# Batch 0's sequence transform by cosine and sine sums, with a compact state and two tables moved

## The reference

```python
# 1. linear attention with decay lam, in blocks of the sequence
intra = (q k^T * Dmask) v ;  inter = (q * lam_pow) kv_state
kv_state = lam_block * kv_state + (k * rev_pow)^T v
# 2. Fourier mixing, normalisation, two-layer network
X = np.fft.fft(np.fft.fft(x, axis=1), axis=2)
u = x + np.real(X)
un = (u - mean(u)) / sqrt(var(u) + 1e-6)
x = u + np.maximum(un @ w_ch1, 0) @ w_ch2
# 3. gated projection
out = (sigmoid(causal_conv5(x)) * (x @ w_val)) @ w_out
```

## Time and profile before

| | us |
|---|---|
| median of three runs | 458.87 (458.79 to 459.09) |
| the profiled execution | 459.72 |
| its span | 457.9 |
| TensorE busy | 438.7 (96%) |
| VectorE busy | 268.2 (59%) |
| ScalarE busy | 151.9 (33%) |
| GpSimd busy | 147.0 (32%) |

### The profile page before, as it was taken

How to read it: one execution, slowest core, us unless ns; L and a number is a source line. 1 busy time by engine, 2 the same in 40 slices (tenths; PEclk the granted TensorE clock), 3 DMA queues, 4 the chain that set the end, 5 groups by cost and what they waited for, 6 DMA issues and landing times.

```text
span 457.9 us, 7070 instructions
## 1 busy us (share of the span) xinstructions
PE 438.7 (96%) x2892; PEld 420.1 (92%) x2892; DVE 268.2 (59%) x419; ACT 151.9 (33%) x284; POOL 147.0 (32%) x99
## 2 busy tenths in 40 slices
PE   6799859999999999999999999999999999999997
PEld 5688749989999999999999999999999999889985
DVE  1657993566835974643533424966565557999220
ACT  1154343065322141111524217344125134525312
POOL 1432536235523222332376422332422450600000
PEclk9899979999999999999999999999999999999999
DMA  6977810050220220202022022022022020001112
GB/s 209 320 219 269 289 67 2 1 183 20 73 94 0 93 77 16 92 1 94 1 93 92 1 92 94 0 93 92 1 92 93 0 93 2 0 1 70 69 47 92
DMA packets 14032, 37.05 MB, mean 81 GB/s; under 512 B 1576, under 2 KB 3120, under 8 KB 14000
## 3 DMA queue, kind: packets, MB, share of 16 engines
q1 hardware_dynamic: 14000, 36.60, 23.8%
HBM read 33.44 MB, written 3.15 MB: 80 GB/s over the span
## 4 chain that ended last, share of the span: by engine, by line
PE 87%; DVE 7%; DMA 3%; ACT 1%; issue 1%; SPq 1%; DVEq 0%
PE ps L550 10%; PE ps L552 9%; PE ps L573 9%; PE ps L572 9%; PE ps L571 9%; PE ps L551 9%; PE ps L489 3%; PE ps L657 2%; PE ps L656 2%; PE ps L655 2%; PE ps L433 2%; PE ps L408 2%; PE ps L634 2%; PE ps L635 2%; PE ps L636 2%; PE ps L444 2%
## 5 line engine op out<-in xcount | busy, mean ns | idle before, releaser
L741 ACT ACTIVATE hh<-ps 128x384 fp32r<-128x384 f32 x64 | 31.5, 492 | 173.1 <-PE ps L552 173.1
L1017 DVE SCALAR_TENSOR_TENSOR hl<-ps,hh 128x384 fp32r<-128x384 f32 x64 | 35.3, 556 | 83.3 <-ACT hh L741 83.3
L550 PE MATMUL ps<-cen_h,w1h_a 128*128 128x384 f32 x128 | 44.1, 344 | 0.5 <-DVE hl L1017 0.5
L550 PE MATMUL ps<-cen_h,w1h_b 128*128 128x384 f32 x128 | 44.2, 345 | 0.0
L552 PE MATMUL ps<-cen_h,w1l_b 128*128 128x384 f32 x128 | 43.1, 337 | 0.0
L552 PE MATMUL ps<-cen_h,w1l_a 128*128 128x384 f32 x128 | 43.1, 337 | 0.0
L573 PE MATMUL ps<-hh,w2l_b 128*128 128x384 f32 x128 | 43.1, 337 | 0.0
L572 PE MATMUL ps<-hl,w2h_b 128*128 128x384 f32 x128 | 43.1, 337 | 0.0
L571 PE MATMUL ps<-hh,w2h_b 128*128 128x384 f32 x128 | 43.1, 337 | 0.0
L551 PE MATMUL ps<-cen_l,w1h_a 128*128 128x384 f32 x128 | 43.1, 337 | 0.0
L551 PE MATMUL ps<-cen_l,w1h_b 128*128 128x384 f32 x128 | 43.0, 336 | 0.0
(11 more groups left out here) (179 smaller groups left out, 1045.5 us busy)
## 6 DMA issues: line engine op xcount, KB each, us to landing
raw_a<-in_mlp SPq DMA_DIRECT2D x16, 512.0 KB, 4.8
raw_b<-in_mlp SPq DMA_DIRECT2D x16, 512.0 KB, 4.4
chunks<-in_qkv SPq DMA_DIRECT2D x12, 512.0 KB, 5.5
chunks<-in_qkv SPq DMA_DIRECT2D x22, 256.0 KB, 4.9
out<-out_sb SPq DMA_DIRECT2D x12, 256.0 KB, 2.0
raw_a<-in_val SPq DMA_DIRECT2D x2, 512.0 KB, 4.5
raw_b<-in_out SPq DMA_DIRECT2D x2, 512.0 KB, 4.6
seq_c<-const_seq SPq DMA_DIRECT2D x1, 768.0 KB, 5.8
```

The costliest lines, as they stand in the source:

```text
L550: mm(bank, wh_, xh, start=r == 0, stop=False)
L741: nc.scalar.activation(hh[:, slot, j], ps[j][:, 0:TB], ACT.Relu).then_inc(s_hh, 1)
L1017: stt(hl[:, slot, j], ps[j][:, 0:TB], 0.0, hh[:, slot, j].bitcast(F32), ALU.max, ALU.subtract).then_inc(s_hl, 1)
```

## The change

Batch 0 takes the same way as batch 1: `seq_tile` and `add_u` go, `seq_pair` and `add_pair` take the batch as an argument. The butterfly's four instructions of `two_pairs` become `two_even` and `two_odd`, and the pieces stand at other chunks. The state holds only its 64x64 blocks, so that `fold_state` is one instruction and `from_state` twice as many, each on a quarter of the array. Hidden transforms 6 and 7 and their radix4 stand among the tiles, 8 and 9 behind the mean, and 10 and 11 in the network's steps. Weight group 0 is loaded at n=3. Its first half is cast at n=3 and subtracted at n=4, the second half after the attention. `mirror(0)` on ScalarE, which waits for the butterfly, stands at n=9 in place of n=8. At the start SP issues only keys and queries of chunk 0 ahead of the powers' write, then the keys, the decay table and the values.

```diff
-            load_chunk(0)
+            load(0, 0, 2, s_tin)
             sp.wait_ge(s_pow, 2 + 7)
             sp.dma_start(rv_dram, rv).then_inc(s_rv, 16)
-            load(1, 0, 2, s_tin)
+            load(0, 2, 3, s_kin)
             sp.wait_ge(s_rv, 16)
             sp.dma_start(decay[:, :, :], ...)
+            load(0, 3, 4, s_vin)
+            load(1, 0, 2, s_tin)
...
                 load_chunk(n)
-                if n == 4:
-                    sp.dma_start(seq_c[:, :], seq_tab[:, 0:LOW_TAB]).then_inc(s_seq, 16)
+                if n == 3:
+                    load_group(0, 0)
                 if n == 5:
-                    sp.dma_start(seq_up[:, :], seq_tab[:, LOW_TAB:]).then_inc(s_seq, 16)
+                    sp.dma_start(seq_c[:, :], seq_tab).then_inc(s_seq, 16)
+                if n == 8:
                     sp.dma_start(cw[:, :, :], conv_w).then_inc(s_cw, 16)
-                if n in (9, 10):
-                    load_group(0, 0, (n - 9,))
```

TensorE:

```diff
                 for hp in range(HP):
-                    mm(out_bank(n)[:, hp * P:(hp + 1) * P], state[:, n % NC % 2, hp, :], qd[:, n % 2, hp, :], ...)
+                    for par in range(2):
+                        rows = slice(par * Dh, (par + 1) * Dh)
+                        mm(out_bank(n)[rows, hp * P:(hp + 1) * P], state[rows, n % NC % 2, hp, :],
+                           qd[rows, n % 2, hp, :], ...)
...
-                if n == N - 2:
-                    seq_tile(3)
                 from_chunk(n)
                 if n == N - 3:
-                    for a in range(R - 1):
-                        seq_tile(a)
+                    seq_pair(0, 0)
+                    seq_pair(0, 1)
+                    hid_transform(NC)
+                if n == N - 2:
+                    seq_pair(0, 2)
+                    hid_transform(NC + 1)
+                    seq_pair(0, 3)
             mean(0)
-            hid_transform(NC)
-            hid_transform(NC + 1)
+            hid_transform(NC + 2)
+            hid_transform(NC + 3)
...
-        HID_AT = {0: (8,), 1: (9, 10), 2: (11,)}
-        RADIX_AT = {0: (9, 10), 1: (11,)}
+        HID_AT = {0: (10,), 1: (11,)}
+        RADIX_AT = {0: (11,)}
```

VectorE, ScalarE and GpSimd:

```diff
                 if n == NC - 1:
                     chunk_pair(0, 0)
+                    chunk_pair(0, 1)
                 if n == NC:
-                    chunk_pair(0, 1)
-                    two_pairs(0)
+                    two_even(0)
                 if n == NC + 1:
+                    two_odd(0)
+                    chunk_pair(0, 2)
+                if n == NC + 2:
                     third_pair(0)
-                if n in (8, 9):
-                    radix4(n - 2)
                 if n == N - 3:
-                    for a in range(R - 1):
-                        add_u(a)
-            add_u(3)
+                    radix4(NC)
+                    add_pair(0, 0)
+                    add_pair(0, 1)
+                if n == N - 2:
+                    radix4(NC + 1)
+                    add_pair(0, 2)
+                    radix4(NC + 2)
+                    add_pair(0, 3)
             hidden_sum(0, 3, nc.vector, dve)
+            radix4(NC + 3)
...
-                if n == 8:
+                if n == 3:
+                    split_group(0, 0)
+                if n == 9:
                     mirror(0)
-                if n == 9:
-                    split_group(0, 0)
-                    split_group(0, 1)
+                    spectrum_copy(NC)
+                if n == 10:
+                    spectrum_copy(NC + 1)
+            split_group(0, 1)
             cen_hi(0, 0)
             cen_hi(0, 1)
-            spectrum_copy(NC)
-            spectrum_copy(NC + 1)
+            spectrum_copy(NC + 2)
+            spectrum_copy(NC + 3)
...
-                if n == 10:
+                if n == 4:
                     split_group(0, 0)
-                    split_group(0, 1)
...
             cen_lo(0)
             cen_lo(1)
+            split_group(0, 1)
```

More of the change, by code:

```diff
@@ L105, in program @@
         w2l_a = sb("w2l_a", [P, 2, R, P], F32R)
[L107 to L111, removed]
+        hh = sb("hh", [P, 2, 2, TB], F32R)
         hl = sb("hl", [P, 2, 2, TB], F32R)
@@ L432, in from_state @@
                 for hp in range(HP):
-                    mm(out_bank(n)[:, hp * P:(hp + 1) * P], state[:, n % NC % 2, hp, :], qd[:, n % 2, hp, :],
-                       start=hp == 0, stop=False, skip_group_check=True)
+                    for par in range(2):
+                        rows = slice(par * Dh, (par + 1) * Dh)
+                        mm(out_bank(n)[rows, hp * P:(hp + 1) * P], state[rows, n % NC % 2, hp, :],
+                           qd[rows, n % 2, hp, :], start=hp == 0, stop=False, skip_group_check=True)
             def from_chunk(n):
@@ L470, in rows_of, with seq_pair @@
                 return (4, 5) if g in (1, 5) else (1, 2)
-            def seq_tile(a):
+            def seq_pair(b, a):
                 if a == 0:
-                    pe.wait_ge(s_r6, R6)
-                    pe.wait_ge(s_seq, 32)
-                if a == 2:
[L478 to L483, removed]
-                        if g % 3 == 0:
-                            mm(o, spectrum(0, g, 0, a), seq_part(g, 0), start=True, stop=False)
-                            m = mm(o, spectrum(0, g, 1, a), seq_part(g, 1), start=False, stop=True)
-                        else:
-                            for i in range(4):
-                                m = mm(o, spectrum(0, rows_of(g)[i % 2], i // 2, a),
-                                       seq_part(g, i), start=i == 0, stop=i == 3)
-                    m.then_inc(s_f, 1)
-            def seq_pair(a):
-                if a == 0:
-                    pe.wait_ge(s_r6, 2 * R6)
-                    pe.wait_ge(s_ye, YE * N)
-                    pe.wait_ge(s_ve, 2)
-                if a == 2:
-                    pe.wait_ge(s_rev, 8)
+                    pe.wait_ge(s_r6, R6 * (b + 1))
+                    if b == 0:
+                        pe.wait_ge(s_seq, 16)
+                    else:
+                        pe.wait_ge(s_ye, YE * N)
+                        pe.wait_ge(s_ve, 2)
+                if a == 2:
+                    pe.wait_ge(s_rev, 4 * (b + 1))
                 for im, bank in ((0, ps[COS]), (1, ps[SIN])):
                     if a:
-                        pe.wait_ge(s_u, added_u(1, a - 1, im))
+                        pe.wait_ge(s_u, added_u(b, a - 1, im))
                     for i, g in enumerate((1, 2)):
@@ L609, in mlp_step @@
                 if 6 <= st.m < 6 + R:
[L610 removed]
+                    seq_pair(1, st.m - 6)
                 if st.m == 10:
@@ L887, in fold_state @@
                     dve.wait_ge(s_pv, n)
-                if n == 0:
-                    dve.wait_ge(s_set, 3)
                 if c:
                     dve.wait_ge(s_sl, HP * (b * (NC - 2) + c))
-                for par in range(2):
-                    rows = slice(par * Dh, (par + 1) * Dh)
-                    new = state[rows, (c + 1) % 2, :, rows]
-                    kv = ps[KV][rows, 0:HP * Dh].rearrange("p (a n) -> p a n", a=HP)
-                    if c:
-                        tt(new, kv, state_l[rows, :, rows], ALU.add).then_inc(s_st, 1)
-                    else:
-                        nc.vector.tensor_copy(new, kv).then_inc(s_st, 1)
+                new, kv = state[:, (c + 1) % 2], ps[KV][:, 0:HP * Dh].rearrange("p (a n) -> p a n", a=HP)
+                if c:
+                    tt(new, kv, state_l[:, :, :], ALU.add).then_inc(s_st, 1)
+                else:
+                    nc.vector.tensor_copy(new, kv).then_inc(s_st, 1)
             def radix4(n):
@@ L1061, in _ @@
             hidden_lo(steps[0])
-            radix4(NC + 2)
+            radix4(NC + 4)
             def taps(b, two, d):
@@ L1112, in mlp_step @@
                     chunk_pair(1, 1)
-                    two_pairs(1)
+                    two_even(1)
+                    two_odd(1)
                 if st.m == 5:
+                    chunk_pair(1, 2)
                     third_pair(1)
@@ L1158, in _ @@
             nc.gpsimd.memset(ones[:, :], 1.0 / D).then_inc(s_set, 1)
-            for i in range(2):
-                nc.gpsimd.memset(state[:, i], 0.0).then_inc(s_set, 1)
             for c in range(B * NC):
```

91 lines of the change are left out of this document (40 added, 51 removed).

## The result

The changed kernel took 451.41 us (median; 450.02 to 452.85), the kernel before 458.98 (458.79 to 459.22): a ratio of 0.9835, with a 95% interval from 0.9803 to 0.9867. That is 7.6 us less; the forecast was 2.2 less, 456.7, with a range from 451.3 to 460.4. Repeated later, the changed kernel took 451.35 against 459.37, ratio 0.9832 [0.9818, 0.9847]. The profiled execution of the changed kernel (450.02, span 448.2) is the fastest of its four, and that of the kernel before (459.72) lies above its median, so the traces differ by 9.7 us where the medians differ by 7.6.

The account below looks back on a forecast made before the run. TensorE bounds until 44, VectorE until 62.7, then TensorE up to the network at 96.62. VectorE's chain -0.3, start +0.6, clock +0.7, transforms -3.2 sum to -2.2 from 458.87: 456.7 us, range 451.3 to 460.4.

Parts of the forecast that it names:

- What bounds the kernel: Attention bound by TensorE until 44, VectorE until 62.7, then TensorE with batch 0's tiles up to the network at 96.62.
- the ledger of VectorE's chain: VectorE's instructions followed in time through butterfly and tiles: the network starts at 96.3, 0.3 us earlier.
- The ledger ahead of the butterfly's end: Butterfly pieces and radix4(5), with VectorE held up by GpSimd's decays: butterfly ends at 67.0, 5.8 us later.
- The ledger from there to the mean: Batch 0's tiles with masks, state and radix4 on VectorE, from 67.0 to the end of the sum at 92.25.
- The later butterfly: Butterfly ending 5.8 us later; 29.3 us from its end to the network in place of 35.4 just pays for it.
- Tiles of batch 0: Four tiles before the mean become bound by VectorE's additions: 13.6 us instead of 17.8.
- Hidden transforms: Fewer stand in the network's steps, which get 3.2 us shorter; the two moved among the tiles cost nothing.
- State: Attention chunks: from_state as 16 quarter products costs 0; fold_state falls from 0.86 us to 0.43 on VectorE.
- Start: New order of the first loads: decay table 1.3 us earlier, bytes ahead of scores(2) 1.9 later, so +0.6 us.
- Clock: Granted clock falls only in the second of two TensorE gaps, ahead of the first tile: +0.7 us.
- Weights: Weight group 0 loaded at n=3, cast and subtracted early on ScalarE and GpSimd: costs nothing.
- The rival with fewer blocks: GpSimd holds up VectorE four times fewer before the tiles: 4.4 us less, 452.3; chance 0.28.

Follow-up runs that it names:

- e8: Changed kernel with GpSimd's decays of keys and queries from chunk 7 on replaced by writes of zeros (decays left out): 445.28 us, ratio 0.9696.
- e7: Changed kernel with the butterfly's pieces back at the chunks where they stood before: 455.14 us, ratio 0.9908.
- e6: Kernel before with the cosine and sine way for batch 0's tiles alone: 453.38 us, ratio 0.9868.
- e10: Changed kernel with hidden transforms 8 and 9 back in the network's steps: 453.49 us, ratio 0.9886.
- e12: Kernel of e9 with radix4 of chunks 7 and 8 moved from VectorE to GpSimd: 447.06 us, ratio 0.9744.
- e5: Kernel before with the compact state alone (fold_state one instruction, from_state 16 quarter products): 459.22 us, ratio 0.9993.
- e4: Kernel before with the new order of loads at the start alone: 458.70 us, ratio 0.9990.
- e1: Changed kernel run again with no edit: 451.35 us.
- e3: Changed kernel with 12 idle products in place of 1 behind scores(0) at the start: 452.28 us, ratio 0.9854.
- e11: Changed kernel with weight group 0 loaded, cast and subtracted at its old places (n=9 and 10): 449.89 us, ratio 0.9794.
- e9: Changed kernel with GpSimd's decays of keys and queries moved out of the butterfly's way by order alone: 447.16 us, ratio 0.9736.

## Why the prediction was right in its direction and wrong in its size

- **What bounds the kernel.** Right: masks ahead of 62.7, tiles behind. Both were where the gain lay.
- **The sum and its error.** The network's first matmul was to come 1.0 us later (-0.3 by the ledger of VectorE's chain, +0.6 start, +0.7 clock). In the two traces it comes 6.3 earlier, at 90.32 in place of 96.62. The 7.3 us between are 2.1 of the ledger ahead of the butterfly's end, 2.6 from there to the mean, 0.2 from the mean on, 1.7 of the start and 0.7 of the clock. The ledger's -0.3 is the term that was mis-sized most. Against the medians the forecast was off by 5.4 us; this pair of traces differs by 2.1 more.
- **The ledger ahead of the butterfly's end.** The mechanism was right: blocks are there, and their time lies on the path (e8). But it ends at 63.8 against 67.0 (67.6 with the start's term). The ledger speaks of eight blocks of about 1.1 us and gives them 7.5 us in its times; the trace has 5.3. The two that are missing stand in radix4(5), which met one block in place of two, because decay_keys(7) started only 0.67 us behind it and not 0.4, and in chunk_pair(0,2), whose last instruction had begun 0.03 us before decay_keys(9). TensorE's wait for radix4(5) was 1.65 us, not 3.2.
- **The ledger from there to the mean.** 22.7 us against 25.3. Of the 2.6, 2.2 are radix4(8): set at 3.3 with a block by GpSimd's sum, it took 1.07, and GpSimd waited for it.
- **The later butterfly** was taken to cost what the rest wins. e7, with the early one, is 3.8 us slower.
- **Tiles of batch 0.** The -4.2 (17.8 us of TensorE's tiles against 13.6 of VectorE's additions) is no term of the sum, which takes the whole chain of VectorE instead. It became e6's expectation, and e6 measures -6.0, of which its trace shows 5.6 between the first tile and the mean. The -4.2 compares the tiles only. When the bound passes from TensorE to VectorE, TensorE's other work in the stretch, 6.2 us of chunks 10 and 11, stops counting as well, and VectorE's mask, state and sum, 3.1, and the first bank's 1.6 begin to count.
- **Hidden transforms.** Forecast 3.2, read 3.4 in the network. e10 shows that the two behind the mean are free there. That transforms 6 and 7 are free among the tiles, as the prediction has it, no run tests by itself, and two readings speak against it: from the first tile to the mean the changed kernel takes 22.6 us and e6, with neither them nor two calls of radix4 between the additions (2.1 us), 18.4; and in e12 TensorE's work, theirs included, is the bound.
- **State.** Forecast 0; e5 can't be told from 0, nor from the 0.4 that its trace shows. The rule of the Trainium skill (TensorEngine Tiling (Array Packing), Key Properties) that a change of tiling mode drains the engine may be what the first hidden product behind the quarters shows, 0.11 us a chunk; the row before could not show it, since no 64x64 form stood there.
- **Start.** Forecast +0.6; e4 excludes that, and shows -0.7 with an interval that reaches to +0.1. The -1.1 of the table lies within what traces of one order differ by. What is seen is that the write of the powers took 1.3 us in place of 3.55, so that the decay table was issued at 4.82 instead of 7.06, 2.2 us earlier and not 1.3. Behind that the bytes did decide: scores(1) waited 4.7 us for chunk 1's load.
- **Clock.** It did not fall in the changed kernel's trace nor in e1's, with a gap of 3.35 us. In e3 and e10 it fell 0.6 and 1.4 us after TensorE had started again behind the same gap, and cost 0.5 and 0.14 us up to the mean; in e11 it fell in the second tile, behind stops of 2.36 and 1.32, and about 1.6 us were lost. The 0.7 of the forecast lies between; no trace here shows the average.
- **Weights.** "Nothing" was not right in its mechanism: the early place let decay_queries(11) run into the butterfly, a block of 0.99. What the place is worth in time stays open (e11).
- The rival with fewer blocks, 452.3, came nearest. It counted four fewer, 4.4 us. The trace has two fewer ahead of the tiles and one in radix4(8), 4.4 us in the ledger's times. Start and clock it had as wrong as the forecast, and they are hidden by the 2.1 us by which the traces differ more than the medians: that it came so near is in part luck.

Of the kernels run that compute everything, e9 and e12 are the fastest, at 447.2 and 447.1, 12 us below the kernel before.

## What to carry to other kernels

When an edit moves the bound of a stretch from one engine to another, sum each engine's whole work in the stretch before and after; the difference of the edited instructions alone misses the work that goes under cover (4.2 expected, 5.6 read and 6.0 measured in e6). Place VectorE's SBUF-to-SBUF work beside GpSimd's idle time, and GpSimd's reads beside VectorE's reads from PSUM: here a mere change of order, with two waits, was worth 4.2 us by the times and 3.3 by the trace. Before moving work off an engine that seems to be the bound, see how long the next engine's own chain is: e12 took 2.1 us from VectorE and won 0.3 in its trace and nothing in its times. And before one trace's reading is called a term, see how much the same stretch differs in the traces of other runs: the start differed by 1.65 us with nothing of it changed.

## What the runs showed of the hardware that was not expected

- A GpSimd instruction whose turn comes between two of VectorE's with two SBUF inputs made the next wait for all of it in the butterfly (1.67 us in place of 0.68), while one that only writes made none wait (0.69). With radix4(8)'s four shorter instructions it did not get between them and waited 0.9 us itself.
- The first group of full-size products behind 64x64 quarters took 0.11 us longer; the quarters themselves run at the pace of half-forms, 16 in 1.02 us.
- After TensorE stopped for 3.35 us the granted clock stayed at full in two traces (after, e1) and fell to half in two others (e3, e10). Up to the mean a fall cost 0.14, 0.5 and 1.6 us (e10, e3, e11), the last when it met a bank that VectorE was about to need.
